# The token layer's two products in plain fp32, with x copied by DMA

## The reference

```python
# attention, q k v: [4, 8, 576, 64]
scores = (q @ k^T) / 8
thresh = max(scores) - tau
scores = where(scores >= thresh, scores, -1e9) - max
attn = exp(scores) / (sum + 1e-9)
x = attn @ v                         # to [4, 576, 512]

# the first mixer layer; its two lines on tokens are the token layer
h = relu(x^T @ w_tok1) @ w_tok2      # w_tok1 [576, 256], w_tok2 [256, 576]
u = x + h^T
y = u + relu(u @ w_ch1) @ w_ch2      # w_ch1 [512, 1536]

# gated convolution layer
h = relu(y @ w_in)
out = (h * sigmoid(conv3(h, conv_w))) @ w_out
```

## Time and profile before

| | |
|---|---|
| median of 3 runs | 849.59 us (848.68 to 851.25) |
| the profiled execution | 850.66 us, its span 848.9 us |
| mean granted clock of TensorE | 0.997 |
| PE busy | 824.3 us, 97% of the span |
| PE, weight loads | 669.5 us, 79% |
| DVE busy | 422.5 us, 50% |
| ACT busy | 412.5 us, 49% |
| POOL busy | 265.7 us, 31% |

### The profile page before, as it was taken

One profiled execution on the slowest core, in us unless ns is written; L12 is line 12 of the kernel. 1 busy time (PEld: TensorE's weight loads), 2 busy tenths in 40 slices (PEclk: granted clock), 3 DMA queues, 4 the chain that ended last, 5 costly groups with the idle time before them and its releaser, 6 DMA issues.

```text
span 848.9 us, 15131 instructions
## 1 busy us (share of the span) xinstructions
PE 824.3 (97%) x5656; PEld 669.5 (79%) x5656; DVE 422.5 (50%) x829; ACT 412.5 (49%) x914; POOL 265.7 (31%) x202
## 2 busy tenths in 40 slices
PE   8999999999999998899999999999999999999998
PEld 4666776767777766788888888888899989898996
DVE  6897878787877774501211211211214819156380
ACT  4887887877878785211211201211114737355461
POOL 0062415142332323470200100120291726428170
PEclk9999999999999999999999999999999999999999
DMA  9311111111111114000000000000320010100101
GB/s 266 111 48 47 48 48 46 46 46 46 46 46 46 50 16 149 1 1 0 1 1 1 0 1 1 1 0 1 128 71 2 1 51 1 45 17 0 49 0 62
DMA packets 20906, 32.70 MB, mean 39 GB/s; under 512 B 4416, under 2 KB 11136, under 8 KB 20864
## 3 DMA queue, kind: packets, MB, share of 16 engines
q1 hardware_dynamic: 20864, 32.13, 11.7%
HBM read 27.41 MB, written 4.72 MB: 38 GB/s over the span
## 4 chain that ended last, share of the span: by engine, by line
PE 84%; DVE 6%; ACT 6%; issue 3%; POOL 0%; ACTq 0%; DVEq 0%; POOLq 0%
PE score L1203 17%; PE score L1318 12%; PE score L999 5%; PE out_t L1218 4%; PE turn_y L1218 4%; PE mixed L1218 4%; PE turn_x L1218 4%; DVE prob L858 4%; PE out_t L1303 4%; PE out_t L1094 4%; PE mixed L1146 3%; PE mixed L1094 3%; PE turn_y L1303 3%; PE mixed L1303 3%; PE turn_x L1303 3%
## 5 line engine op out<-in xcount | busy, mean ns | idle before, releaser
L921 DVE SCALAR_TENSOR_TENSOR h<-score,h 128x512 fp32r<-128x512 f32 (+1 forms) x60 | 38.3, 638 | 243.5 <-ACT h L693 243.5
L693 ACT ACTIVATE h<-score 128x512 fp32r<-128x512 f32 (+1 forms) x60 | 33.3, 555 | 250.5 <-PE score L1203 250.5
L841 DVE TENSOR_SCALAR_CACHE_REDUCE negs<-score,neg_scale 128x576 f32<-128x576 f32 x144 | 112.7, 816 | 58.7 <-PE score L999 34.0
L858 DVE SCALAR_TENSOR_TENSOR prob<-negs,thresh,exps 128x576 f32<-128x576 f32 x144 | 134.2, 964 | 0.3 <-ACT thresh L594 0.3
L591 ACT ACTIVATE exps<-negs,neg_max 128x576 f32<-128x576 f32 x144 | 104.6, 772 | 1.9 <-DVE negs L841 1.5
L999 PE MATMUL score<-qk 64*128 64x288 f32 x512 | 85.5, 434 | 1.6 <-DVE negs L841 1.0
L1203 PE MATMUL score<-uh,w1h 128*128 128x512 f32 (+1 forms) x240 | 86.9, 368 | 0.0
L1203 PE MATMUL score<-uh,w1l 128*128 128x512 f32 (+1 forms) x240 | 86.8, 368 | 0.0
L1203 PE MATMUL score<-ul,w1h 128*128 128x512 f32 (+1 forms) x240 | 86.8, 368 | 0.0
L559 POOL TENSOR_TENSOR zl<-z,zh 128x512 fp32r<-128x512 f32 x32 | 54.2, 1694 | 98.7 <-ACT zh_t L779 98.7
L999 PEld LDWEIGHTS score<-qk 64*128 64x128 f32 x512 | 46.9, 188 | 28.0 <-issue 13.1
(11 more groups left out here) (184 smaller groups left out, 2010.0 us busy)
## 6 DMA issues: line engine op xcount, KB each, us to landing
qk<-in_qk SPq DMA_DIRECT2D x16, 640.0 KB, 3.9
vm<-in_v SPq DMA_DIRECT2D x16, 320.0 KB, 4.2
result<-ostage SPq DMA_DIRECT2D x16, 256.0 KB, 2.1
w1f<-in_moe_w_ch SPq DMA_DIRECT2D x4, 768.0 KB, 10.8
w2f<-in_moe_w_ch SPq DMA_DIRECT2D x4, 768.0 KB, 7.4
wif<-in_moe_w_in SPq DMA_DIRECT2D x1, 2048.0 KB, 7.8
wof<-in_moe_w_out SPq DMA_DIRECT2D x8, 256.0 KB, 2.6
wt2f<-in_moe_w_tok SPq DMA_DIRECT2D x1, 576.0 KB, 9.4
```

The source lines that it names most:

```text
L841: nc.vector.tensor_scalar(negs[:, i, h, :].rearrange("p (c s) -> p c s", c=2), raw_of[h], neg_scale[:, 0:1], None, ALU.mult, ALU.min, accu ...
L858: nc.vector.scalar_tensor_tensor(out=prob[:, i, h * S:(h + 1) * S], in0=negs[:, i, h, :], scalar=thresh[:, i, h:h + 1], in1=exps[i][:, h, ...
L921: nc.vector.scalar_tensor_tensor(out=h3[:, n % RING, 1, 0:w], in0=hidden_banks[n % 4][:, 0:w], scalar=0.0, in1=h3[:, n % RING, 0, 0:w].bit ...
```

## The change

Both products of the token layer are computed with fp32 matmuls on unsplit operands: five matmuls in place of 15 in `mix_hidden`, two in place of six in each group of `mix_out`. The parts xh, xl, h1h, h1l, wt1h, wt1l, wt2h, wt2l and POOL's operations that made them are gone, and ACT drains the hidden tile once. `xs`, the buffer of two pairs, is filled by a DMA on SP's queue (`copy_x`), once x is complete and, in odd bodies, once both hidden groups have read the buffer. All that waited for `x_split` waits for `x_copied`. PE waits for the weights' loads in place of their split.

```diff
--- before.py
+++ after.py
-    xh = x_parts.put("xh", [P, NT, 2 * P], F32R)
-    xl = x_parts.put("xl", [P, NT, 2 * P], F32R)
+    xs = x_pairs.put("xs", [P, NT, 2 * P])
...
+            def copy_x(at):
+                pair = at.g - 1
+                mine = slice((at.k - 1) % 2 * P, (at.k - 1) % 2 * P + P)
+                sp.wait_ge(x_done, pair + 1)
+                sp.wait_ge(short_x, pair + 1)
+                if at.hid:
+                    sp.wait_ge(tok_done, at.g - 1)
+                sp.dma_start(xs[:, :, mine], x32[:, :, :]).then_inc(x_copied, DMA)
...
                 if 1 <= k < PAIRS - 1:
                     sp.wait_ge(pv_done, g)
                     load_v(g + 1, 1 - par)
+                if at.pv:
+                    copy_x(at)
...
-            def split_x(at):
...
-                copy(xh[:, :, mine], x32[:, :, :]).then_inc(xs_hi, 1)
...
-                nc.gpsimd.tensor_tensor(xl[:, :, mine], x32[:, :, :], xh[:, :, mine].bitcast(F32), ALU.subtract) \
-                    .then_inc(x_split, 1)
...
-            def rest_of_token(at, i):
...
-            def split_wt(kts):
...
                 if at.mix:
                     add_u(g - 4)
-                for i in range(KT if at.hid else 0):
-                    rest_of_token(at, i)
-                if at.pv:
-                    split_x(at)
                 if at.mix:
                     add_u(g - 3)
-                if k == 1:
-                    split_wt(range(NT))
...
-                nc.scalar.activation(h1h[:, i, :], mixed[:, 0:2 * P], ACT.Relu).then_inc(hid_hi, 1)
-                nc.scalar.activation(h1f[:, i, :], mixed[:, 0:2 * P], ACT.Relu).then_inc(hid_left, 1)
+                nc.scalar.activation(h1[:, i, :], mixed[:, 0:2 * P], ACT.Relu).then_inc(hid_left, 1)
...
                 if k >= 1:
-                    act.wait_ge(x_split, pair)
+                    act.wait_ge(x_copied, DMA * pair)
...
                 if k >= 1:
-                    dve.wait_ge(x_split, pair)
+                    dve.wait_ge(x_copied, DMA * pair)
...
-                        pe.wait_ge(wt_split, NT + KT)
-                    pe.wait_ge(x_split, g - 1)
+                        pe.wait_ge(wt_loaded, 3 * DMA)
+                        pe.wait_ge(set_once, 2)
+                    pe.wait_ge(x_copied, DMA * (g - 1))
...
                 for kt in range(NT):
-                    for wt, x in ((wt1h, xh), (wt1l, xh), (wt1h, xl)):
-                        mm = nc.tensor.matmul(mixed[:, 0:2 * P], wt[:, kt, i * P:(i + 1) * P], x[:, kt, :],
-                                              start=(n == 0), stop=(n == 3 * NT - 1))
-                        n += 1
+                    mm = nc.tensor.matmul(mixed[:, 0:2 * P], wt1[:, kt, i * P:(i + 1) * P], xs[:, kt, :],
+                                          start=(kt == 0), stop=(kt == NT - 1))
...
-                    pe.wait_ge(tok_lo, g - 2)
+                    pe.wait_ge(hid_left, g - 2)
...
                     for kt in range(KT):
-                        for h, wt in ((h1h, wt2h), (h1h, wt2l), (h1l, wt2h)):
-                            mm = nc.tensor.matmul(bank[:, 0:HALF], h[:, kt, i * P:(i + 1) * P],
...
+                        mm = nc.tensor.matmul(bank[:, 0:HALF], h1[:, kt, i * P:(i + 1) * P],
+                                              wt2[:, kt, c * HALF:(c + 1) * HALF],
+                                              start=(kt == 0), stop=(kt == KT - 1))
```

More of the change, by code:

```diff
@@ L92, in build @@
     W1_EARLY = 7
-    x_parts = Region(w1l_at - 2 * size([P, NT, 2 * P]))
-    xh = x_parts.put("xh", [P, NT, 2 * P], F32R)
-    xl = x_parts.put("xl", [P, NT, 2 * P], F32R)
-    assert x_parts.at == w1l_at and w1l_at - 2 * size([P, NT, 2 * P]) >= fixed.at + W1_EARLY * size([P, KM, P])
+    x_pairs = Region(w1l_at - size([P, NT, 2 * P]))
+    xs = x_pairs.put("xs", [P, NT, 2 * P])
+    assert x_pairs.at == w1l_at and w1l_at - size([P, NT, 2 * P]) >= fixed.at + W1_EARLY * size([P, KM, P])
     w2l_at = ch1.at
@@ L135, in build @@
     x32 = s1.put("x32", [P, NT, P])
-    h1f = s1.put("h1f", [P, KT, 2 * P])
+    h1 = s1.put("h1", [P, KT, 2 * P])
     u_part = s1.put("u_part", [P, S])
[L138 to L147, removed]
+    wt1 = s1.put("wt1", [P, NT, DT])
+    wt2 = s1.put("wt2", [P, KT, S])
     s2 = Region(w2l_at)
@@ L241, in build @@
         short_x = sem("short_x")
-        x_split = sem("x_split")
+        x_copied = sem("x_copied")
         xt_done = sem("xt_done")
@@ L245, in build @@
         xt_tail_drained = sem("xt_tail_drained")
-        hid_hi = sem("hid_hi")
         hid_left = sem("hid_left")
-        wt_split = sem("wt_split")
         tok_done = sem("tok_done")
-        tok_lo = sem("tok_lo")
         u_done = sem("u_done")
@@ L373, in load_wt @@
             def load_wt():
-                sp.dma_start(wt1f[:, 0:FULL, :], w_tok1[0:MAIN, :].rearrange("(t p) n -> p t n", p=P)) \
+                sp.dma_start(wt1[:, 0:FULL, :], w_tok1[0:MAIN, :].rearrange("(t p) n -> p t n", p=P)) \
                     .then_inc(wt_loaded, DMA)
-                sp.dma_start(wt1f[0:TAIL, FULL, :], w_tok1[MAIN:S, :]).then_inc(wt_loaded, DMA)
-                sp.dma_start(wt2f[:, :, :], w_tok2.rearrange("(t p) n -> p t n", p=P)).then_inc(wt_loaded, DMA)
+                sp.dma_start(wt1[0:TAIL, FULL, :], w_tok1[MAIN:S, :]).then_inc(wt_loaded, DMA)
+                sp.dma_start(wt2[:, :, :], w_tok2.rearrange("(t p) n -> p t n", p=P)).then_inc(wt_loaded, DMA)
+            def copy_x(at):
[6 more added lines that the diff above has]
+                sp.dma_start(xs[:, :, mine], x32[:, :, :]).then_inc(x_copied, DMA)
             load_qk(0, 0)
@@ L507, in split_u @@
                 op.then_inc(u_lo, 1)
-            pool.wait_ge(set_once, 2)
-            def split_wt(kts):
[L512 to L515, removed]
             def body(at):
@@ L520, in body @@
                     add_u(g - 4)
-                for i in range(KT if at.hid else 0):
-                    rest_of_token(at, i)
-                if at.pv:
-                    split_x(at)
                 if at.mix:
                     add_u(g - 3)
-                if k == 1:
-                    split_wt(range(NT))
-                if k == 2:
-                    for kt in range(KT):
-                        split_weight(wt2h[:, kt, :], wt2l[:, kt, :], wt2f[:, kt, :], wt_split)
                 if k % 2 == 1 and k < 2 * W1_EARLY:
@@ L828, in _ @@
             nc.vector.memset(x32[TAIL:P, FULL, :], 0.0).then_inc(set_once, 1)
-            nc.vector.memset(wt1f[TAIL:P, FULL, :], 0.0).then_inc(set_once, 1)
+            nc.vector.memset(wt1[TAIL:P, FULL, :], 0.0).then_inc(set_once, 1)
             dve.wait_ge(tau_used, 2)
@@ L1171, in mix_out @@
                         pe.wait_ge(xt_drained, g)
-                    n = 0
                     for kt in range(KT):
-                        for h, wt in ((h1h, wt2h), (h1h, wt2l), (h1l, wt2h)):
-                            mm = nc.tensor.matmul(bank[:, 0:HALF], h[:, kt, i * P:(i + 1) * P],
-                                                  wt[:, kt, c * HALF:(c + 1) * HALF],
-                                                  start=(n == 0), stop=(n == 3 * KT - 1))
-                            n += 1
+                        mm = nc.tensor.matmul(bank[:, 0:HALF], h1[:, kt, i * P:(i + 1) * P],
+                                              wt2[:, kt, c * HALF:(c + 1) * HALF],
+                                              start=(kt == 0), stop=(kt == KT - 1))
                     mm.then_inc(u_done, 1)
```

11 lines of the change are left out of this document (removed).

## The result

The changed kernel takes 857.34 us, the median of five runs (855.66 to 858.58), against 849.59 before: +7.75 us, a ratio of 1.0087 with an interval of 1.0072 to 1.0102. It is slower, where 853.0 was forecast with the chance on that side. But the step is more than twice the +3.4 forecast, and 857.34 is close to what the second rival, the one with two masks held by each chunk of w1, was priced at (856.8). The profiled execution has a span of 855.5 us at a mean granted clock of 0.997, so 6.6 us over the span before; the other 1.1 us are there because the execution profiled before lay that far above its median.

A forecast was written before the change was run, and what follows sets the result against it. PE was taken as the bound, busy 824 of 848.9 us. Terms 6.0 + 2.9 - 3.2 - 1.8 + 1.75 - 1.4 - 0.8 = +3.45 us gave 849.6 + 3.4 = 853.0 us, range 847.8 to 857.5.

The forecast's parts named there:

- the second rival: In the loop, each of five w1 chunks holds two masks, 5.5 us in place of 1.75: 856.8 us, chance 0.15.
- Part 4: POOL's w1 chunks move behind the even body's second add and hold masks: +1.75 us, from 0.5 to 5.5.
- the two cases: At a moved chunk: w1h alone holds a mask, 0.1 us lost, or w1h and w1l hold one each, 1.1 us.
- Part 3: POOL's splits go and DVE's masks get faster: -3.2 us in six even bodies, -1.8 us in bodies 1 and 2.
- my case: The add delays the first mask, so the moved chunk most likely meets only the second: 0.35 us a chunk.
- Part 1: Hidden product in odd bodies, five fp32 matmuls for 15 fp32r: +0.37 us a group, +6.0 us, nothing hidden.
- Part 2: Output product, two fp32 matmuls for six fp32r: +0.17 us a group, partly hidden in even bodies, +2.9 us.
- The rival of a farther relief: Faster masks save more in the loop's bodies than credited, so the change is no slower: chance 0.3.
- Part 5: End of the attention stage, shorter PE waits in k = 15 (-0.3) and k = 17 (-1.1): together -1.4 us.
- Part 6: PE's half-clock stretch at 66 to 70 us may vanish with body 2's slow masks: -0.8 us, between 0 and -1.7.
- Part 7: Sixteen DMA copies of x on SP's queue, each landing in about 4 us, cost nothing; w2's later loads neither.

The follow-up runs named there:

- the chunk alone: The kernel before, with only the loop's chunks of w1 issued one body earlier, right behind the even body's second add: 852.54 us, ratio 1.003.
- useless splits: The changed kernel plus two POOL operations nobody reads, between the two adds of u in the loop's five even bodies: 852.53 us, ratio 1.0043.
- the window for w1: The changed kernel, with each chunk of w1 on POOL waiting until the masks of its own body are done: 849.36 us, ratio 1.0002.
- the relief alone: The changed kernel's structure with 15 and 6 fp32r matmuls per group again, on once-rounded operands without low parts: 850.7 us, ratio 1.0002.
- the copy on POOL: The changed kernel, with x copied by one POOL operation at the old split's place instead of by DMA: 851.06 us, ratio 1.0012.
- the first chunks: The changed kernel, with only the w1 chunks of k = 1 and 3 waiting for the masks of their body: 855.61 us, ratio 1.0065.
- both lessons: The kernel before, all splits kept, with POOL's w1 chunks moved behind their body's masks and odd bodies' x splits behind the next body's first two: 844.67 us.
- the matmuls alone: The kernel before, with one fp32 matmul on the high parts replacing each three fp32r ones, POOL's splits and waits kept: 858.26 us, ratio 1.0098.

## Why the prediction was wrong in size

**Part 4 failed, the moved chunk.** It had 0.35 us for each of five chunks and nothing for the first two. Measured were 1.06 and, for the two together, 0.8: 6.1 us in place of 1.75, as much as the whole miss (4.35). The price I had worked out for two masks held, 1.1 us, was right to 0.04; what failed was the choice between the two cases. I chose by where the second add stood in the trace of before, over the first mask. But that trace had a split of x ahead of the add, and part 3 of the same prediction took this split away. The add moved up by the 0.7 us that decided which of POOL and DVE came first. The run with the chunk alone (0.52) shows that my case does come up while the splits are there, and the run with useless splits (0.22) that it comes back with them. For the first two chunks I had the wrong body: they start at 25.10 us, in body 0 and not in body 1, and there DVE goes from eviction to mask and on with almost no pause, so that PE pays for a held mask.

The Trainium skill (SBUF — State Buffer, Who interferes with whom) calls the pair of ports that DVE and GpSimd share an exclusive lock. It adds that a DVE instruction with at most one SBUF input, outside the modes that use both pairs, stays out of it, and that the order of issue decides which engine waits. The traces agree: the scores' eviction keeps its 0.82 us beside the add, the mask of 0.81 us takes 1.47 when w1h starts ahead of it, and w1h takes 1.57 in place of 1.04 when the mask is first. A held mask ends 0.6 us after POOL's operation, though, and not the full 0.82 that it takes alone.

**Part 1, right per group, a little dear per body.** A group takes 2.16 us as scaled by columns. "Nothing of it hidden" was wrong by 0.2 us in each odd body of the loop; taken for the bodies up to 13 that is an estimated 1.3 us in all.

**Part 2 held.** 0.97 us a group, +0.34 in an even body for 0.32. Its bounds were added up wrongly: 0.17 and 0.68 in the six bodies give 2.0 and 5.1 us, not 2.2 and 4.9. Nothing hangs on it.

**Part 3 held.** 0.66 us an even body for 0.53, so -4.0 for -3.2. Bodies 1 and 2 are 0.4 and 1.2 us shorter once the first chunks are out of the way, -1.6 for -1.8. The rival of a farther relief did not come true; it credits 5.5 us more than I did, and the bodies show 0.6 more (0.8 in the even ones, less 0.2 in bodies 1 and 2).

**Part 5 held.** PE's wait for ACT's copy in k = 15 is 0.56 us in place of 0.84. The wait at the end of k = 17 is 0.47 us in place of 1.61 and ends with ACT's one copy:

```profile
360.46 1.24 PE L1130 MATMUL out_t<-wt,h 128*128 128x288 f32 x4 [0.47 <-ACT h L610]
...
365.88 0.50 PE L1172 MATMUL out_t<-h,w2h 128*128 128x512 f32 x1 [0.50 <-ACT u_part L632]
```

The first projection waits for ACT as before, so w2, issued behind the copies, was in time. It was later than I had worked out, though: DVE takes its first quarter 15 us later than before, not 8, and waits 9 us for it.

```profile
350.50 0.96 DVE L897 CAST w2h<-w2f 128x1536 fp32r<-128x1536 f32 x1 [9.03 <-DMA w2f<-in_moe_w_ch]
```

From body 15's tail transpose to the first projection it is 53.91 us for 51.08, of which some 1.7 is a stretch of half clock; the 1.1 left is what parts 1, 2 and 5 make of these bodies.

**Part 6 failed.** The half clock at 66 us is gone with the slow masks there, but another is in the same profile at 324.3 us, behind a wait of PE in body 15. The kernel before has the same wait, of 0.9 us in both, and no half clock behind it. The mean clock is 0.997 in both. A spread would have been right here, and no term of the sum.

**Part 7 held.** 2.8 us for the 4 taken, and no wait on it.

Summed against the profiled execution: 6.1 for part 4's 1.75, 0 for part 6's -0.8, less 1.3 (part 1) and 0.6 (part 3), give 3.45 + 4.35 + 0.8 - 1.9 = 6.7, and 6.7 was measured (857.34 less 850.66), closer than the parts are known. The rival's price came within 0.6 us partly by luck: it had nothing for the first chunks (0.8) and kept part 6's -0.8, and parts 1 and 3, too dear by 1.9 together, made up for both. The range held by under 0.2 us, because it took the rival in, and the rival deserved more than 0.15: its own argument ("w1h would be queued the moment the add ends, and a mask is due then") needed only the add's new time.

## What to carry to other kernels

When a change removes an operation from a queue, all that stood behind it in that queue starts earlier; place each of those against the other engines anew, at its new time, before costing it. Where two engines shut each other out, 0.2 us decides who comes first, and the price of an operation is then set by where it stands and not by how long it is: 72 us less work on POOL won 5.6 us at the masks that it had held, and lost 6.1 at others that what was left then came to hold. In the kernel before nearly the same work, moved by a few us, won 4.4. Give an engine's spare work an explicit window, by a wait on the event after which the other engine leaves the resource alone, and don't let it start where the queue happens to be free.

## What the runs showed of the hardware

An fp32 matmul of 256 columns takes 0.43 us with the full array (ten records, 2.16 us for five), to three fp32r ones at 0.36: one fp32 product costs a fifth more than the three fp32r ones that split it. At 288 columns it is 0.485 to 0.40, the same ratio.

The clock falls behind a stretch in which PE waited, but not behind each. Windows of the changed kernel (busy us of PE, PEld, DVE, ACT, POOL, then the granted clock, DMA share, GB/s), and its hidden group in the third:

```profile
66.00:70.00 4.00, 4.00 (x46) 2.56 (x42) 2.91 (x7) 2.68 (x7) 0.00 (x0) 1.00 0.01 2
...
320.00:324.00 4.00, 2.75 (x39) 1.86 (x38) 3.13 (x8) 3.56 (x12) 0.00 (x0) 1.00 0.02 4
324.00:328.00 4.00, 4.00 (x14) 3.17 (x12) 0.99 (x3) 0.70 (x2) 0.00 (x0) 0.57 0.01 2
```

```profile
324.27 4.01 PE L1104 MATMUL mixed<-xs,wt 128*128 128x256 f32 x10
```

The same place of the program in the run with the window for w1:

```profile
313.70:317.70 4.00, 2.75 (x39) 1.82 (x38) 3.13 (x8) 3.56 (x12) 0.00 (x0) 1.00 0.02 4
317.70:321.70 4.00, 4.00 (x31) 3.32 (x31) 0.99 (x3) 2.07 (x8) 0.00 (x0) 1.00 0.01 2
```

PE is busy for 2.75 of four microseconds in both, in body 15. In one profile some 3.4 us at 1.2 GHz follow, in which the group takes 4.01 us for 2.32 elsewhere, and in the other nothing. Leaving out the last few us of the program, the ten profiles have eleven such stretches of 3.4 us, each within some 2 us of waits of PE that add up to 0.8 us or more. The wait in body 15 (0.9 us) is in all ten; the half clock follows it in six of them, at 314 to 324 us: the changed kernel, the relief alone, the copy on POOL, the chunk alone, the first chunks and both lessons. The stretch at 65 to 67 us is in the kernel before, the matmuls alone and the chunk alone, all three with slow masks in body 2; one at 30 us is in the relief alone and one at 46 us in the chunk alone. The run with the window and that with the useless splits have none. One such stretch costs 1.6 to 1.7 us. In the changed kernel's five runs the time goes with the mean clock, 855.66 us at 1.0 and 858.58 at 0.995; that is why the table has the fastest run of each kernel. What decides between one execution and the next stays open; no run here was made for it.
